# Token mixing inside the first quad, and the splits of the weights dealt out anew, in a three-layer float32 kernel

## What is computed

```python
def _moe_ref(x, w_tok1, w_tok2, w_ch1, w_ch2):         # x: 2 x 768 x 512
    xt = x.transpose(0, 2, 1)
    h = np.maximum(xt @ w_tok1, 0.0) @ w_tok2           # token mixing: 768 -> 256 -> 768
    u = x + h.transpose(0, 2, 1)
    h2 = np.maximum(u @ w_ch1, 0.0) @ w_ch2             # channel mixing: 512 -> 1536 -> 512
    return u + h2

def _moe2_ref(x, mu_k, mu_r, w_k, w_v, w_r):
    x_prev = np.concatenate([np.zeros((B, 1, D)), x[:, :-1, :]], axis=1)
    xk = mu_k * x + (1.0 - mu_k) * x_prev
    xr = mu_r * x + (1.0 - mu_r) * x_prev
    k = np.maximum(xk @ w_k, 0.0)                       # 512 -> 1024
    v = k * k @ w_v
    return 1.0 / (1.0 + np.exp(-(xr @ w_r))) * v
```

## Time and profile before

| | us |
|---|---|
| median of 3 runs | 509.62 |
| lowest and highest | 506.69, 512.02 |
| the profiled execution | 508.96 |
| its span in the trace | 507.1 |
| PE busy in that span | 472.7 (93%) |
| DVE, ACT, POOL busy | 288.6, 223.3, 184.9 |

### The profile page before, as it was taken

One profiled execution on the slowest core, in us unless ns is written; L12 is line 12 of the kernel. 1 busy time (PEld: TensorE's weight loads), 2 busy tenths in 40 slices (PEclk: granted clock), 3 DMA queues, 4 the chain that ended last, 5 costly groups with the idle time before them and its releaser, 6 DMA issues.

```text
span 507.1 us, 8294 instructions
## 1 busy us (share of the span) xinstructions
PE 472.7 (93%) x2896; PEld 425.3 (84%) x2896; DVE 288.6 (57%) x654; ACT 223.3 (44%) x470; POOL 184.9 (36%) x163
## 2 busy tenths in 40 slices
PE   4788899999879999998799999998999999999996
PEld 4677778788879999897799999997889989989985
DVE  4688797486645553555656467578346355454521
ACT  3888797466222433422223343224355255353411
POOL 5454464256465444654745352595000000000000
PEclk9999899999989999999799999998999999999999
DMA  9899998110211212212223122130010001001001
GB/s 199 179 204 213 224 208 192 39 41 1 83 43 42 85 49 77 83 43 83 84 83 122 45 84 85 42 126 1 1 41 21 0 21 41 0 0 62 0 0 62
DMA packets 53466, 38.11 MB, mean 75 GB/s; under 512 B 21441, under 2 KB 45761, under 8 KB 53441
## 3 DMA queue, kind: packets, MB, share of 16 engines
q1 hardware_dynamic: 53440, 37.78, 29.1%
HBM read 33.43 MB, written 3.15 MB: 72 GB/s over the span
## 4 chain that ended last, share of the span: by engine, by line
PE 80%; DVE 6%; DMA 4%; issue 3%; ACT 3%; POOL 2%; SPq 2%; DVEq 0%; ACTq 0%; POOLq 0%
PE bank L1131 18%; PE bank L1132 18%; PE bank L1133 18%; PE bank L1264 13%; PE bank L1265 6%; DMA kn<-in_k_dram 3%; DMA v<-in_v_dram 2%; PE bank L1183 2%; PE bank L1161 1%; SPq L357 1%; PE bank L1113 1%; PE bank L1080 1%; PE bank L1202 1%; ACT e_sb L634 1%; DVE rL L1012 1%
## 5 line engine op out<-in xcount | busy, mean ns | idle before, releaser
L1131 PE MATMUL bank<-ucH,w1H 128*128 128x384 f32 x168 | 58.1, 346 | 9.8 <-DVE c L1007 9.6
L1132 PE MATMUL bank<-ucL,w1H 128*128 128x384 f32 x168 | 57.2, 341 | 0.0
L1133 PE MATMUL bank<-ucH,w1L 128*128 128x384 f32 x168 | 57.2, 340 | 0.0
L748 ACT ACTIVATE rH<-c 128x384 fp32r<-128x384 f32 x36 | 18.9, 526 | 76.5 <-DVE c L1007 76.5
L1131 PE MATMUL bank<-xkH,WkH 128*128 128x384 f32 x128 | 43.6, 341 | 2.0 <-DVE k L1056 2.0
L1131 PEld LDWEIGHTS bank<-ucH,w1H 128*128 128x128 f32 x168 | 32.4, 193 | 14.7 <-issue 11.4
L1133 PE MATMUL bank<-xkH,WkL 128*128 128x384 f32 x128 | 43.8, 342 | 0.0
L1132 PE MATMUL bank<-xkL,WkH 128*128 128x384 f32 x128 | 43.6, 341 | 0.0
L1056 DVE SCALAR_TENSOR_TENSOR k<-bank,kr 128x384 f32<-128x384 f32 x32 | 17.8, 555 | 36.4 <-ACT kr L778 36.4
L1264 PE MATMUL bank<-rL,w2H 128*128 128x512 f32 x96 | 38.1, 397 | 0.0
L1264 PE MATMUL bank<-rH,w2L 128*128 128x512 f32 x96 | 38.1, 397 | 0.0
(11 more groups left out here) (142 smaller groups left out, 1264.5 us busy)
## 6 DMA issues: line engine op xcount, KB each, us to landing
...
```

Of the source, the lines that this page charges most:

```text
L748: act.activation(rH[slot][:, f, half * GR:half * GR + GR], src, ACT.Relu).then_inc(rh_done, 1)
L1131: pe.matmul(dst, wH, mH, start=start, stop=False, **more)
L1132: pe.matmul(dst, wH, mL, start=False, stop=False, **more)
L1133: return pe.matmul(dst, wL, mH, start=False, stop=stop, **more)
```

## The change

1. Token mixing's second half. Tiles 8 to 15 (batch 1) no longer stand ahead of quad 0, but inside it, in the gaps between its products, where later quads have the second layer's chunks. The order on PE is now tiles 0 to 7, `h1` of batch 1, quad 0 with tiles 8 to 15. `h1` of batch 1 moves from banks 0 and 1 to banks 6 and 7. `h1`, `w2H` and `w2L` are laid out batch by batch, so that `w_ch2`'s first piece can be written when tile 7 is done. ACT's and DVE's work on `w_ch1`'s first piece and on the combinations of batch 0 is spread over tiles 3 to 7 and the time of `h1`.
2. Combinations for batch 1 (`T_AHEAD`, `U_AHEAD`) start one quad later, with two in quad 2 and two in quad 4.
3. The low parts of all pieces that pass through stage 2 move from POOL to DVE (`low_piece`): for `w_ch2` in every quad between R22 and `c21`, for the three pieces of the last layer between R21 and `c12`. These three now stand in quads 7, 8 and 9 instead of 6, 7 and 8.
4. Residual adds of batch 0 are parted into `wide` and `side` and stand at other places between quad 6's sums; quad 6 has the same `GAPS` as the others.
5. The seven pieces of `TAIL` are split by ACT (`high_tail`) and DVE (`low_tail`): three at once behind quad 11, the others behind f = 0, 3, 5 and 6 of the last layer's first group, which stands ahead of the loop for it.

The diff, cut to its core:

```diff
-        U_AHEAD = ((0,), (1,), (2,), (3,), (4, 6), (5,))
-        T_AHEAD = ((3,), (4,), (6,), (5,))
+        U_AHEAD = ((), (0,), (1, 2), (3,), (4, 6), (5,))
+        T_AHEAD = ((), (3,), (4,), (6,), (5,))
...
-        SLOT2 = [("w2", n) for n in range(NFP + 1)]
-        SLOT2 += [("wk", 0), ("w2", NFP + 1), ("wk", 1), ("w2", NFP + 2), ("wv", 0)]
-        SLOT2 += [("w2", n) for n in range(NFP + 3, NQ)]
+        SLOT2 = [("w2", n) for n in range(NFP + 2)]
+        SLOT2 += [("wk", 0), ("w2", NFP + 2), ("wk", 1), ("w2", NFP + 3), ("wv", 0)]
+        SLOT2 += [("w2", n) for n in range(NFP + 4, NQ)]
...
+        TAIL_FIRST, TAIL_AFTER = TAIL[0:3], {0: TAIL[3], 3: TAIL[4], 5: TAIL[5], 6: TAIL[6]}
...
         @block.sync
+                elif m == 2:
+                    sp.wait_ge(wb_split, len(SLOT2))
                 else:
-                    sp.wait_ge(wb_split, len(SLOT2) + (m - NSTG + 1 if m >= NSTG else 0))
+                    sp.wait_ge(tail_split, m - NSTG + 1)
...
         @block.gpsimd
...
             def split(kind, n):
-                m = split_count(kind, n)
                 slot, landed = stage_of(kind, n)
-                hi, lo = split_dst(kind, n)
+                hi = split_dst(kind, n)[0]
                 pool.wait_ge(ld_w[slot], landed)
                 pool.tensor_copy(hi, stg[slot][:, :]).then_inc(wb_high, 1)
-                pool.wait_ge(wb_high, m)
-                pool.tensor_tensor(lo, stg[slot][:, :], hi.bitcast(F32), ALU.subtract).then_inc(wb_split, 1)
 
...
-            pool.wait_ge(tok2_done, NGR * KT)
-            pool.wait_ge(u_done, NGR * KT)
             for q in range(NQ):
                 if 1 <= q < NQ - 1:
                     sums_w1(q + 1)
+                if q < 2:
+                    pool.wait_ge(tok2_done, 2 * KT * (q + 1))
                 wait_second(pool, q - 2)
                 split("w2", q)
+                if q == 1:
+                    pool.wait_ge(u_done, NGR * KT)
                 if q < len(T_AHEAD):
                     for i in T_AHEAD[q]:
                         combine_u(1, i)
@@ -593,11 +601,6 @@
                     if SLOT2[n][0] != "w2" and SLOT2[n - 1] == ("w2", q):
                         pool.wait_ge(prod_done, NPROD * NFP)
                         split(*SLOT2[n])
-            pool.wait_ge(prod_done, NPROD * NQ)
-            for kind, n in TAIL:
-                if (kind, n) == ("wv", 1):
-                    pool.wait_ge(rl_done, 4 * NQ)
-                split(kind, n)
...
         @block.scalar
...
+                slot, landed = stage_of(kind, n)
+                act.wait_ge(ld_w[slot], landed)
+                act.activation(split_dst(kind, n)[0], stg[slot][:, :], ACT.Copy).then_inc(tail_high, 1)
+
...
-                if n == KT - 1:
+            for n in range(2 * KT):
+                turn_out_x(n)
+                if n == 3:
                     high_w1(0)
+                elif n == 5:
                     act.wait_ge(u_done, KT)
                     high_u(0, 0)
+                elif n == 6:
                     high_u(0, 1)
-                    high_w1(1)
-                    high_h1(2)
-                    high_h1(3)
-                if n == 2 * KT:
-                    act.wait_ge(u_done, 2 * KT)
-                if n - 2 * KT in (0, 1, 2, 4, 5):
-                    high_u(0, U_ORDER[(2, 3, 4, None, 5, 6)[n - 2 * KT]])
-            act.wait_ge(u_done, NGR * KT)
+            act.wait_ge(u_done, 2 * KT)
+            high_u(0, 2)
+            high_u(0, 3)
+            high_u(0, 4)
+            high_h1(2)
+            high_u(0, 6)
+            high_u(0, 5)
+            high_h1(3)
...
             def quad(q):
...
                 act.wait_ge(prod_done, done + P1)
                 act.activation(p1[:, :], bank[0][:, 0:GR], ACT.Copy).then_inc(p1_done, 1)
+                turn_out(0, 1)
                 act.wait_ge(prod_done, done + P2)
                 wait_second(act, q - 2)
                 high_r(R11, 0, 0, bank[0][:, 0:GR])
-                if 1 <= q < NQ - 1:
+                turn_out(2, 3)
+                if q < NQ - 1:
                     high_w1(q + 1)
                 act.wait_ge(sum_done, 5 * q + 3)
                 high_r(R22, 1, 1, c22[:, :])
+                turn_out(4)
                 act.wait_ge(sum_done, 5 * q + 4)
                 high_r(R21, 1, 0, c21[:, :])
+                turn_out(5)
                 if q < NFP:
                     for i in U_AHEAD[q]:
                         high_u(1, i)
                 act.wait_ge(sum_done, 5 * q + 5)
                 high_r(R12, 0, 1, c12[:, :])
+                turn_out(6, 7)
...
         @block.vector
...
+            def low_piece(kind, n):
+                hi, lo = split_dst(kind, n)
+                dve.wait_ge(wb_high, SLOT2.index((kind, n)) + 1)
+                dve.tensor_tensor(lo, stg[2][:, :], hi.bitcast(F32), ALU.subtract).then_inc(wb_split, 1)
+
+            def low_tail(kind, n):
+                hi, lo = split_dst(kind, n)
+                dve.wait_ge(tail_high, TAIL.index((kind, n)) + 1)
+                dve.tensor_tensor(lo, stg[stage_of(kind, n)[0]][:, :], hi.bitcast(F32),
+                                  ALU.subtract).then_inc(tail_split, 1)
+
+            for n in range(2 * KT):
+                add_x(n)
+                if n == 3:
                     low_w1(0, 0)
+                elif n == 4:
                     low_w1(0, 1)
+                elif n == 5:
                     low_u(0, 0)
+                elif n == 6:
                     low_u(0, 1)
-                    low_w1(1, 0)
-                    low_w1(1, 1)
-                    low_h1(2)
-                    low_h1(3)
-                if n - 2 * KT in (1, 2, 3, 5, 6):
-                    low_u(0, U_ORDER[(None, 2, 3, 4, None, 5, 6)[n - 2 * KT]])
+            low_u(0, 2)
+            low_u(0, 3)
+            low_h1(2)
+            low_u(0, 4)
+            low_u(0, 6)
+            low_u(0, 5)
+            low_h1(3)
...
             def quad(q):
...
+                add(0)
                 plus(P6, u2, Bk, p1)
+                add(1)
                 low_r(R11, 0, 0, A)
+                add(2)
                 plus(P7, u3, Bk, p1)
-                if 1 <= q < NQ - 1:
+                if q < NQ - 1:
                     low_w1(q + 1, 0)
-                if q == NFP:
-                    residual(0, 0)
+                add(3)
                 dve.wait_ge(sum_done, 5 * q + 2)
                 if q:
                     dve.wait_ge(rl_done, 4 * q)
                 plus(P5, c22, A, u3)
                 low_r(R22, 1, 1, c22[:, :])
+                low_piece("w2", q)
+                add(4)
                 if q == NFP:
-                    residual(0, 1)
+                    wide(0, 0)
                 plus(P4, c21, Bk, p1)
-                if 1 <= q < NQ - 1:
+                if q < NQ - 1:
                     low_w1(q + 1, 1)
                 low_r(R21, 1, 0, c21[:, :])
+                add(5)
+                for n in range(1, len(SLOT2)):
+                    if SLOT2[n][0] != "w2" and SLOT2[n - 1] == ("w2", q):
+                        low_piece(*SLOT2[n])
+                if q == NFP:
+                    wide(0, 1)
                 for i in ahead:
                     low_u(1, i)
+                plus(P3, c12, A, u2)
                 if q == NFP:
-                    residual(0, 2)
-                plus(P3, c12, A, u2)
+                    side(0, 1)
                 low_r(R12, 0, 1, c12[:, :])
+                add(6, 7)
                 if q == NFP:
-                    residual(0, 3)
+                    wide(0, 2)
+                    wide(0, 3)
+                    side(0, 3)
                 if q in MIXED_AFTER:
                     mixed(0, 0, xkH, xkL, MIXED_AFTER[q])
 
             for q in range(NQ):
                 quad(q)
+            for kind, n in TAIL_FIRST:
+                low_tail(kind, n)
             for d in range(KT):
-                residual(1, d)
+                wide(1, d)
+                if d % 2:
+                    side(1, d)
             dve.wait_ge(x2_done, 6 * B)
 
...
         @block.tensor
...
+            for n in range(2 * KT):
+                token(n)
+            hidden_tiles([(n, st) for n in range(TT, 2 * TT) for st in range(ST)])
...
-            GAPS, GAPS_LAST = (1, 1, 1, 1, 1, 1, 2), (2, 2, 2, 1, 1, 0, 0)
+            GAPS = (range(0, 1), range(1, 2), range(2, 3), range(3, 4), range(4, 5), range(5, 6), range(6, 8))
             for q in range(NQ):
-                todo = list(CHUNKS) if q else []
                 for n in range(NPROD):
                     product(q, n)
-                    for _ in range((GAPS_LAST if q == NFP else GAPS)[n] if q else 0):
-                        second(q - 1, *todo.pop(0))
+                    for m in GAPS[n]:
+                        if q:
+                            second(q - 1, *CHUNKS[m])
+                        else:
+                            token(2 * KT + m)
             for f, d in CHUNKS:
```

143 lines of the change are left out of this document (82 added, 61 removed).

## The result

The changed kernel takes 529.32 us (median of 4 runs, 526.93 to 531.66), the kernel before in the same comparison 508.15 (4 runs, 505.89 to 512.02). The ratio is 1.042 (95% interval 1.036 to 1.048): slower by over 4%. The forecast was 511.6 with a range to 519, and it was wrong. The profiled execution after took 528.7 us, its span 527.0, against 507.1 before: 19.9 us more.

A forecast was written before the change was run, and what follows sets the result against it. PE, busy 93% of the span, was taken as the floor, so only its stalls and half clock could be won. Gains 5.2 + 6.7 + 3.7 = 15.6, losses 3.2 + 14.4 = 17.6, net 2.0 us slower: 511.6 us, range 503 to 519.

The forecast's parts named there:

- Tiles 8 to 15 inside quad 0: Front and quad 0: tiles fill PE's waits between products; gain of 5.2 us, bounds 2 and 7.1.
- tile 8 waits about 0.2 us for `h1`'s last low part: Cost counted inside quad 0: PE's tile 8 held about 0.2 us by h1's last low part.
- quad 0 doesn't fill: Rival, quad 0: late adds of tiles 8 to 15 take back 3 to 4 us, plus clock, 516 us; chance 0.13.
- Low parts of w_ch2 on DVE: Quads 1 to 5: DVE's added low parts delay c12; loss of 3.2 us, bounds 1.5 and 7.
- what follows is later by about 0.8 us: Every quad: w_ch2's low part ahead of c21 makes DVE's following steps about 0.8 us later.
- The second rival: DVE and GpSimd hold each other up, 0.6 us in each of nine quads plus slow clock: 520 us; chance 0.22.
- Three pieces of the last layer: Quads 7 to 9: reload of stage 2 delays c12; three times 4.8 us, loss of 14.4, bounds 9.3 and 17.
- The chain: Quads 7 to 9: stage 2 load, GpSimd's copy, DVE's low part, then c12; stalls PE 3.1 us.
- The first rival: The wait in quads 7 to 9 is short, most of the 14.4 us doesn't come; 506.5 or 497 us; chance 0.2.
- Quad 6: Quads 6 and 7: common GAPS cut the stall before quad 7 to 0.7 us; gain 6.7, bounds 5 and 7.4.
- Tail: Last layer's first group: with GpSimd silent the 2.01 us stall and its slow clock go; gain 3.7, bounds 4 and 0.

The follow-up runs named there:

- Experiment 10: Changed kernel with last-layer low parts and GpSimd's sums behind c12, h1's last low part before three low_u, GpSimd's first w_ch2 split after those: 497.08 us.
- experiment 5: Experiment 2's kernel with h1's last high and low parts moved ahead, and GpSimd's first w_ch2 split kept until VectorE's low_u are done: 493.99 us.
- experiment 6: Experiment 2's kernel with only VectorE's and ScalarE's order changed, h1's last parts moved ahead; GpSimd splits w_ch2's first piece at once: 495.54 us.
- Experiment 3: Changed kernel with GpSimd's four sums for the next quad starting only when c12 is made, not when P3 has ended: 516.43 us.
- Experiment 1: Changed kernel with VectorE's low parts of WkL0, WkL1 and WvL0 behind c12 and R12's low part instead of ahead of c12: 511.52 us.
- experiment 7: Experiment 2's kernel with quad 6 undone (residual adds and GAPS_LAST as in the kernel before): 507.58 us.
- experiment 8: Experiment 2's kernel with the seven last pieces split by GpSimd alone, as in the kernel before: 505.96 us.
- experiment 2: Changed kernel with the low parts of all stage 2 pieces made by GpSimd again, the rest unchanged: 502.38 us.
- experiment 11: Experiment 5's kernel with GpSimd's sums starting only behind c12: 491.71 us.

## Why the prediction was wrong, step by step

**Tiles 8 to 15 inside quad 0: forecast a gain of 5.2, measured a loss of 1.0** (2.35 up to quad 2, less the stall of 1.37 before it, which belongs to the next part). Apart from tile 8 the front ran nearly without waits (0.69 us for the first chunk, 0.45 and 0.26 at two tiles), and there was no stall before quad 1, as forecast. The step that failed is "tile 8 waits about 0.2 us for `h1`'s last low part". It waited 3.66 us, and the clock over that stretch was 0.93, which is 0.07 x 25.1 = 1.8 us: together 5.3 of the 6.2 us missed here. The 0.2 had no row behind it. It leaves out two things that GpSimd does to this order: its instructions stretch the three `low_u` ahead of the low part from about 2.7 to 4.58 us, and its last combination holds up the `high_u` behind which ScalarE makes `h1`'s high part. The kernel before had shown the first: between its tiles two `low_u` took 1.70 and 2.13 us (from 121.67 and 123.76) beside GpSimd's combinations. Experiment 10 shows the size, 4.8 us for a stall as long as here, and experiments 5 and 6 the same with a longer one. The rival "quad 0 doesn't fill" placed its trouble at the adds, where there was next to none.

**Low parts of w_ch2 on DVE: forecast a loss of 3.2 us, measured 12.4** (11.0 from P1 of quad 2 to that of quad 6, and the 1.37 before quad 2). The step that failed is "what follows is later by about 0.8 us", with the steps that follow priced as if GpSimd were silent. Here the mechanism that I had made a rival is the cause: with 0.8 us more work ahead of it, VectorE's last `low_r` and `low_u` meet GpSimd's four sums, which begin when P3 ends. Experiment 3 shows it directly, since it changes only when these sums start: the stalls fall near the prediction's numbers. The second rival's size, 0.6 us per quad, was too small as well. It was taken from one `low_r`; the `low_u` behind it lose another 1.1 us in a quad with two of them, and the stalls of 2.77 us brought half clock in quads 3 and 5. The kernel before had that row as well, right behind the one in the earlier trace rows; with GpSimd silent a `low_u` takes 0.87 to 0.95:

```profile
140.11 1.47 DVE L955 TENSOR_TENSOR ucL<-u,ucH 128x768 fp32r<-128x768 f32 x1
```

My argument against the rival, that in quad 3 VectorE's chain ran at its own pace beside the same sums, looked at VectorE alone. GpSimd's first sum there, before:

```profile
188.95 1.50 POOL L543 TENSOR_TENSOR w1S<-stg 128x256 f32<-128x256 f32 x1 [6.32 <-PE bank L1133]
```

VectorE's `low_u` had started at 188.89, 0.06 us ahead, and it was the sum that took 1.50 us in place of 0.73. The two did meet, and GpSimd paid; 0.8 us later it was VectorE. A chain that wins such a meeting by a hair is no evidence that the two get along.

The Trainium skill, "SBUF — State Buffer", section "Who interferes with whom", says which steps are exposed: those with two inputs in SBUF (the memory of all tiles outside the banks), when GpSimd's instruction reads SBUF too, while a step with at most one, outside VectorE's two-port modes, is not. Row by row the trace agrees: `low_u`, `low_r` of `c21` and the low part of a last-layer piece lengthen beside GpSimd, `c12` and `low_h1` keep 0.55 and 0.68 us. I had quoted the first half of this rule in the prediction and given the rival 0.22; by rule and rows together it deserved most of the weight.

**Three pieces of the last layer: forecast 14.4 us, measured 17.4** (quads 8 to 10 are 13.7 us longer than before, and the 3.74 us before quad 8). The chain was right to the instruction. Stalls of 3.74, 3.72 and 3.77 us (11.2) against 3.1 each (9.3), and half clock of 2.7, 1.5 and 1.3 us (5.5) against 1.7 each (5.1). The mis-sized terms are the piece's low part, 1.73 us for 1.22, again beside GpSimd's sums, and the load, 3.56 for 3.34. Experiment 1 takes back 17.8, some of it by chance. The first rival, that these waits are short, is refuted.

**Quad 6: forecast 6.7, measured 5.9** (quads 6 and 7 took 38.8 us before, and 36.7 after with the 3.74 us that belong to the pieces), and 5.2 by experiment 7. In the kernel after, a stall of 1.15 us was left where 0.7 was forecast; with GpSimd's sums out of the way it is 0.61 (experiment 3).

**Tail: forecast 3.7, measured 3.7** in the profile and 3.6 by experiment 8. The mixing steps lost their delay as soon as GpSimd was silent.

So two terms of five failed, by 6.2 and 9.2 us, one was 3.0 short and one 0.8 too large; with the 1.3 us of the attention part against them these make the 17.9 us by which the span was missed. The first three have one origin in common: VectorE's steps were priced at the length that they have while GpSimd leaves them alone, and in the front ScalarE's wait for GpSimd came on top. Of the 26.9 us that the low parts cost (experiment 2), about 5.4 are the work itself (experiments 10 and 11), and the rest is what it waits for and what ran beside it.
